# Key values of both streams in one slot, decay products of round 0 in another order, first steps on VectorE

## The reference

```
state = 0                                   # per batch and head, 48 x 48
for t in range(768):
    y[t]  = r[t] @ (state + (u * k[t]) outer v[t])
    state = w[t][:, None] * state + k[t] outer v[t]
x = y as [3072 tokens, 384]
x = (x @ w_a) * (x @ w_b) @ w_out           # 384 -> 1536 -> 384
h = x @ w_in                                # 384 -> 2048
out = (max(h, 0) + alpha * min(h, 0)) @ w_out2
```

## Time and profile before

| | |
|---|---|
| median of 3 runs | 1026.67 us |
| lowest, highest | 1026.21, 1026.68 us |
| the profiled execution | 1026.15 us |
| its span | 1024.4 us |
| busy: PE, DVE, ACT, POOL | 98%, 55%, 28%, 3% |
| granted clock of TensorE | 1.00 in every slice |

### The profile page before, as it was taken

How to read it: one execution, slowest core, us unless ns; L and a number is a source line. 1 busy time by engine, 2 the same in 40 slices (tenths; PEclk the granted TensorE clock), 3 DMA queues, 4 the chain that set the end, 5 groups by cost and what they waited for, 6 DMA issues and landing times.

```text
span 1024.4 us, 29087 instructions
## 1 busy us (share of the span) xinstructions
PE 1001.1 (98%) x12448; PEld 975.5 (95%) x12448; DVE 561.9 (55%) x1166; ACT 288.4 (28%) x604; POOL 30.2 (3%) x28
## 2 busy tenths in 40 slices
PE   5899999999999999999999999999999999999998
PEld 4789999999999999999999999999999999999998
DVE  7587664655646646556432436655454555545554
ACT  3435324224232142241222434222222222122211
POOL 4500200000000000000000000000000000000000
PEclk9999999999999999999999999999999999999999
DMA  6454231311213113020020313010101010101000
GB/s 183 110 158 115 63 81 30 95 42 38 85 30 79 37 30 91 4 61 28 25 60 1 107 64 121 4 47 1 47 1 47 1 46 0 46 0 47 8 17 24
DMA packets 42167, 53.01 MB, mean 52 GB/s; under 512 B 5184, under 2 KB 42048, under 8 KB 42048
## 3 DMA queue, kind: packets, MB, share of 16 engines
q1 hardware_dynamic: 40624, 51.04, 17.6%
q10 hardware_dynamic: 1424, 0.23, 0.2%
HBM read 39.46 MB, written 9.44 MB: 48 GB/s over the span
## 4 chain that ended last, share of the span: by engine, by line
PE 95%; DVE 2%; issue 1%; ACT 1%; DMA 1%; ACTq 0%; SPq 0%; DVEq 0%
PE products L166 17%; PE products L168 16%; PE products L167 16%; PE acc L166 11%; PE acc L168 11%; PE acc L167 11%; PE products L697 6%; PE products L712 1%; PE products L741 1%; PE products L757 1%; PE products L674 1%; PE products L726 1%; DVE f_y L920 1%; DMA w_v<-in_w_dram 1%; DVE k_in L932 0%
## 5 line engine op out<-in xcount | busy, mean ns | idle before, releaser
L166 PE MATMUL products<-x_parts,weights_hi 128*128 128x384 f32 x576 | 200.9, 349 | 2.2 <-DMA x_parts<-f_y 0.5
L167 PE MATMUL products<-x_parts,weights_hi 128*128 128x384 f32 x576 | 194.1, 337 | 0.0
L168 PE MATMUL products<-x_parts,weights_lo 128*128 128x384 f32 x576 | 193.9, 337 | 0.0
L1232 DVE TENSOR_SCALAR leaky_low<-products,leaky_al 128x384 f32<-128x384 f32 x128 | 79.0, 618 | 169.4 <-PE products L168 169.3
L1092 DVE TENSOR_TENSOR g_sb<-a_g,products 128x384 f32<-128x384 f32 x96 | 53.2, 554 | 192.7 <-issue 134.2
L1179 ACT ACTIVATE leaky_g_hi<-leaky_g_sb 128x384 fp32r<-128x384 f32 x128 | 67.3, 526 | 295.0 <-DVE leaky_g_sb L1237 295.0
L515 ACT ACTIVATE g_hi<-g_sb 128x384 fp32r<-128x384 f32 x96 | 50.3, 524 | 259.6 <-DVE g_sb L1092 259.6
L166 PEld LDWEIGHTS products<-x_parts,weights_hi 128*128 128x128 f32 x576 | 108.0, 188 | 7.4 <-issue 3.8
L168 PEld LDWEIGHTS products<-x_parts,weights_lo 128*128 128x128 f32 x576 | 108.2, 188 | 0.0
L167 PEld LDWEIGHTS products<-x_parts,weights_hi 128*128 128x128 f32 x576 | 108.2, 188 | 0.0
L166 PE MATMUL acc<-g_hi,weights_hi 128*128 128x384 f32 x288 | 97.7, 339 | 1.6 <-DVE g_lo L1098 1.0
(11 more groups left out here) (86 smaller groups left out, 1761.9 us busy)
## 6 DMA issues: line engine op xcount, KB each, us to landing
k_in<-in_k_dram SPq DMA_DIRECT2D x16, 336.0 KB, 4.1
r_in<-in_r_dram SPq DMA_DIRECT2D x16, 336.0 KB, 5.8
stage<-in_w_out_dram SPq DMA_DIRECT2D x14, 384.0 KB, 3.2
w_v<-in_v_dram SPq DMA_DIRECT2D x16, 288.0 KB, 4.0
y_dram<-x_in SPq DMA_DIRECT2D x8, 576.0 KB, 3.1
x_in<-y_dram SPq DMA_DIRECT2D x8, 576.0 KB, 4.6
out_dram<-leaky_out_sb SPq DMA_DIRECT2D x7, 576.0 KB, 3.3
stage<-in_w_dram SPq DMA_DIRECT2D x10, 336.0 KB, 4.0
```

Of the source, the lines that this page charges most:

```text
L166: pe.matmul(out, w_hi, x_hi, start=first, stop=False)
L167: pe.matmul(out, w_hi, x_lo, start=False, stop=False)
L168: return pe.matmul(out, w_lo, x_hi, start=False, stop=last)
L1232: dve.tensor_scalar(self.low[f % 2][:, :], h, 0.0, self.al[:, f:f + 1], ALU.min, ALU.mult).then_inc(self.low_ready, 1)
```

## The change

- The key values of both streams are made in the slot of phase 8; phase 9 has no slot; the weighted values of stream 0 go to the slot of phase 10. `slot_at` and `shared_bank` are changed to match: at phase 9 `up_b` has bank 0 or 1 and waits until the states of stream 0 are carried; at phase 10 the order stays `up_a`, `down`, `up_b`.
- In round 0, VectorE makes the decay products of level 2 ahead of the second leaf merge, and the step of stream 1's keys at level 2 ahead of the decay products of levels 3 to 6.
- The first steps of round 2 go from POOL to VectorE, behind the leaf merges; those of round 1 stay on VectorE but go behind `g_sb` and `g_lo` of piece 0. SP loads the decays of round 2 ahead of moving the rows of round 1's output.
- Weight piece 5 is split at g = 1 with piece 6, not at g = 0.

```
-FIRST_NEW = [5, 6, 7, 9, 10, 11, 13, 15, 16, 17, 18, 18, 18]
+FIRST_NEW = [5, 5, 7, 9, 10, 11, 13, 15, 16, 17, 18, 18, 18]
...
 def slot_at(g):
-    return g >= 0 and step_at(g) is not None and step_at(g) % PHASES != 1
+    return g >= 0 and step_at(g) is not None and step_at(g) % PHASES not in (1, 9)
 def shared_bank(g):
-    return slot_at(g - 1) and slot_at(g)
+    return slot_at(g) and (slot_at(g - 1) or step_at(g) % PHASES == 10)
...
                     elif phase == 10:
-                        move_last_unit(n)
+                        if n == 0:
+                            move_last_unit(n)
                         if n + 1 < STAGED_FROM:
                             load_w(n + 1, 0)
                             load_w(n + 1, 1)
+                        if n > 0:
+                            move_last_unit(n)
...
@@ gpsimd: the function first_step_k is removed, and
-                for n in range(2, STAGED_FROM):
-                    for j in range(2):
-                        first_step_k(n, j)
-                        step_r(n, j, 0)
...
@@ tensor: attend
                     elif phase == 8:
                         key_values(n, 0)
-                    elif phase == 9:
                         key_values(n, 1)
+                    elif phase == 10:
                         weighted_values(n, 0)
-                    elif phase == 10:
                         outputs(n)
@@ tensor: up_b
+                    elif step_at(g) % PHASES == 9:
+                        pe.wait_ge(states_done[0], states_after(step_at(g) // PHASES))
                     elif not shared_bank(g):
                         pe.wait_ge(merged, merges(step_at(g) // PHASES, 0, g % 2))
@@ tensor: the loop over g
-                    if slot_at(g - 1):
+                    down_first = slot_at(g - 1) or shared_bank(g)
+                    if down_first:
                         down(g - 1)
                     if g > 0:
                         up_b(g)
-                    if g > 0 and not slot_at(g - 1):
+                    if g > 0 and not down_first:
                         down(g - 1)
@@ vector: attend
+                def first_steps(n):
+                    for j in range(2):
+                        first_step_k(n, j)
+                        step_r(n, j, 0)
...
                     if phase == 0 and n > 0:
                         for j in range(2):
                             merge_leaf(n, j)
-                        if n == 1:
-                            for j in range(2):
-                                first_step_k(n, j)
-                                step_r(n, j, 0)
+                        if n == 2:
+                            first_steps(n)
...
                     elif phase == 1 and n > 0:
+                        if n == 1:
+                            first_steps(n)
                         products_of_w(n, 0, 2, range(1, 7))
@@ vector: round 0
                 products_of_w(0, 1, 1, (1,))
+                products_of_w(0, 0, 2, (2,))
                 merge_leaf(0, 1)
                 step_k(0, 1, 1)
+                step_k(0, 0, 2)
                 merge_level(0, 0, 1)
                 merge_level(0, 1, 1)
-                products_of_w(0, 0, 2, (2,))
-                step_k(0, 0, 2)
+                step_k(0, 1, 2)
                 products_of_w(0, 0, 2, range(3, 7))
-                for step in range(3, BEFORE_TILES):
-                    if step > 3:
-                        attend_early(step)
+                merge_level(0, 0, 2)
+                merge_level(0, 1, 2)
+                for step in range(4, BEFORE_TILES):
+                    attend_early(step)
                     attend(step)
```

More of the change, by code:

```diff
@@ L481, in step_r @@
                     pool.tensor_tensor(halves(t, h, 1), halves(t, h, 1), decay(n, j, h, 0), ALU.mult).then_inc(r_stepped[j], 1)
-                def first_step_k(n, j):
-                    pool.wait_ge(w_loaded[j], 16 * (n + 1))
-                    pool.wait_ge(k_prepared[j], n + 1)
-                    pool.tensor_tensor(halves(k_in[j], 1, 0), halves(k_in[j], 1, 0), decay(n, j, 1, 1), ALU.mult).then_inc(k_first[j], 1)
                 def last_step_k(n, j):
```

## The result

The changed kernel takes 1029.59 us (median of 18 runs, 1027.76 to 1032.36), the kernel before 1026.68 in the same series (18 runs, 1025.02 to 1027.84). The ratio is 1.0031, 95% interval [1.0023, 1.0039]: 0.3% slower, where 0.3% faster was forecast. The profiled execution of the change took 1032.01 us with a span of 1030.2, near the upper end of its runs; about 2.4 us of it belong to this execution and not to the median.

What follows compares the result with a forecast made beforehand. TensorE, 95% of the chain that ended last, was taken as the bound. Terms 3.1 - 3.85 + 1.0 + 0.9 + 1.9 = 3.0 us gained gave a median of 1023.7 us, range 1022.2 to 1025.2.

Steps and rivals of the forecast that it cites:

- A: Rounds 1 to 7: one slot less saves switches and idle time on TensorE; 3.1 us gained, bounds 2.4 and 3.4.
- B: Rounds 1 to 7, phase 9: `down` newly waits for `g_lo`, 0.55 us a round; 3.85 us lost.
- C: Piece 0: `g_sb` starts sooner, so `down` no longer leaves TensorE idle; 1.0 us gained, bounds 0.3 and 1.5.
- D: Round 2: first steps off POOL no longer delay VectorE, so `down` doesn't wait; 0.9 us gained, bounds 0.4 and 1.1.
- the second rival: Piece 8 late or VectorE's two splits holding TensorE longer: C is 0.3 or nothing, time 1024.5 us; chance 0.08.
- E: Round 0: reordered decay products and key step shorten TensorE's key waits; 1.9 us gained, bounds 0.4 and 2.6.
- The first: Rival in the front: work moved ahead runs at TensorE's slow pace, losing 1.0 to 1.3 us; time 1024.9; chance 0.20.
- one of the signs that the prediction names: Sign of a wrong forecast: in round 0, the state products of stream 1 run at the slow pace.
- The third: Rival in rounds 1 to 7: the new wait B doesn't appear, time 1019.8 us; chance 0.05.
- The fourth: Rival: `up_b` of phase 9 waits because VectorE carries stream 0's states late; time 1030.7 us; chance 0.05.

Runs made afterwards that it cites:

- run 1: The kernel before with the slot part of the change alone: 1031.33 us against 1026.68, ratio 1.0043.
- run 3: The kernel before with the first steps of rounds 1 and 2 moved and piece 5 split at g = 1, nothing else: 1025.59 us, ratio 0.9984.
- run 2: The kernel before with the new order of VectorE's work in round 0 alone: 1024.62 us, ratio 0.9984.
- run 4: The changed kernel with its slot part undone, so new front order and first steps together: 1024.46 us, ratio 0.9981 to the kernel before.
- run 5: The changed kernel with 96 more instructions, turned keys of stream 0 computed twice in round 1: 1026.82 us, ratio 1.0004 to the kernel before.
- run 6: The changed kernel with 48 more instructions, half of stream 0's turned keys computed twice in round 1: 1027.78 us against 1026.1, ratio 1.0017.
- run 9: The kernel of run 4 with both streams' key values in slot 8 and stream 0's weighted values in slot 9: 1021.99 us, ratio 0.996 to the kernel before.
- run 10: The changed kernel with stream 0's weighted values between `up_a` and `down` of the phase 10 piece: 1021.06 us, ratio 0.9944 to the kernel before.
- run 7: The kernel before with the leaf products of rounds 2 to 7 computed twice, a burst of 384 instructions: 1041.1 us, ratio 1.0139.

## Why the prediction was wrong

**A, one slot less, 3.1 gained: right as far as it went.** Slot 8 lasts 1.21 us. Where nothing stops, slots 8 to 10 together take 0.34 us (odd) and 0.41 (even) less, and one entry of 0.10 is gone: 3.3. But A also said that the weighted values "cost the same in slot 10 as in 9". **This is the step that failed.** It costed a longer burst at its matmuls alone and the supply of instructions at nothing. In slot 10 the 96 added instructions brought the burst across a second block boundary in three of seven rounds, at 1.41, 1.22 and 1.26 us by the rows, 3.9 in all (4.6 from start to start, in an execution 2.4 us over the median). A - B was forecast at -0.75 for the slots; run 1 measured -4.65, and 3.9 is the difference, in which the slower clock behind a stop may have its part too.

**B, a new wait, 3.85 lost: right**, in place, count and size: seven waits, 0.3 idle by the row, 0.56 a round, 3.9.

**C, piece 0, 1.0 gained, and D, round 2, 0.9 gained.** D: the wait for `x_in` of 0.67 us is gone. The 0.9 of D is there whole in run 3, and nothing of C is. C: the gain at piece 0 was there and was lost again within four pieces. VectorE's two splits made TensorE wait 0.43 for `g_sb`, as the sum allowed for, and piece 8, loaded behind four transfers, held ScalarE by 1.14 us. TensorE's timeline of the change, and ScalarE's:

```profile
65.93 0.41 PE L166 MATMUL products<-x_parts,weights_hi 128*128 128x384 f32 x1 [0.43 <-DVE g_sb L1095]
...
68.22 0.85 ACT L138 ACTIVATE weights_hi<-stage 128x768 fp32r<-128x768 f32 x1 [1.14 <-DMA stage<-in_w_out_dram]
```

That is the second rival, held unlikely because the piece is used only at g = 4. It is staged earlier, and the engine that stages it also serves TensorE. Run 3 gives C and D together 1.1 to 1.6 instead of 1.9.

**E, round 0, 1.9 gained: right by itself** (1.6 to 2.1 in run 2). In the seven other traces with the new order the first big matmul starts at 42.87 to 45.05 us, in the change at 47.83: there E is outweighed by the stop of 3.70 us and by the slot with the state products, which takes 1.6 us longer than before. How much of that is in the median can't be read from one trace.

**The rivals.** The first (E given back by the pace) happened in part: the slot of round 0 with the state products, 5.59 us before, took 4.94 to 6.23 in the seven other kernels with the new order and 7.21 in the change, where stream 1 ran at the slow pace, one of the signs that the prediction names. What sets the moment of the faster pace stays open; the granted clock reads 1.00 throughout. The third (no wait B) is refuted. The fourth, slower because states come late, came near to the measured time with a wrong mechanism: `products` never waits for `state` at phase 9. That stops for issue were in the profile before, the 0.41 above among them, in a stream that had just such bursts, was the hint that I passed over: I looked at what each engine waited for, and took "issue" for no cost of the change's.

By the medians: +0.75 for A and B as forecast, +3.9 for the stops and -2.0 for C, D and E together (run 4; forecast -3.8) is +2.7; measured +2.9. So about two thirds of the error is the stops, perhaps with a slower clock behind them, and the rest is that C, D and E gave half of their forecast together, C nothing of it. One open end: runs 5, 6, 9 and 10 are each some 0.7 to 2 us faster than these parts add up to. Run 4 may have measured C, D and E too low (its interval reaches from 0.8 to 3.2 us gained), or the change may lose in its front too.

## What to carry to other kernels

Where an engine runs bursts of very short instructions, count them as instructions and not only as time. Behind the front and but for one stop beside heavy DMA traffic, no burst stopped here that did not span two block boundaries, and two bursts of 96 and 288 with large matmuls between cost nothing where one of 384 stopped for over a microsecond. Read an "issue" wait in the middle of a run of like instructions as a price that an edit can move, and shift the stream by some instructions to see whether it is one. When work is moved away from a place, look whether it had covered a chain there: splitting the burst gave back the cover and the supply at once.

## What the runs showed of the hardware

- TensorE's instructions come in packets of 16 KB, 256 instructions. In slot 10 and the leaf bursts the packet of a block started 0.6 to 1.2 us after the block before had been entered, and TensorE went on 1.2 to 1.7 us after the packet's end, 3.0 to 3.7 us after that entering. At some 7.3 ns an instruction a block lasts 1.9 us, so the second boundary within a burst cost 0.84 to 1.66 us by the rows, in fourteen of fourteen bursts whose first boundary was 52 instructions or more inside and the second inside too. Where the DMA engines were busy the packet started up to 5.8 us after the entering (the stops of 0.76 and 3.70 us).
- A boundary at 4 to 19 instructions into the burst did no harm: the next packet had started 1.7 to 1.9 us before TensorE's turn at that boundary, while the big matmuls ahead of the burst still ran.
- After stops of 1.66, 1.58 and 0.76 us the granted clock fell to means of 0.62 to 0.69 over 4 to 5 us, with big matmuls at 0.32 us instead of 0.175; after the stops of 1.22 to 1.41 us in the change and of 0.92 and 0.90 in run 7 it stayed at 1.00. A stop can so cost more than its length, and its length does not tell when; what does is open.
